# Undilated attention heads in blocks of 32 queries by 64 keys instead of 48 by 80, in a kernel of windowed attention and two feed-forward stages

## The reference, cut to what matters

```
scores = scale * q @ k.T                                   # B=4, H=8, S=576, D=64
mask_plain = (rel >= 0) & (rel < 32)                       # heads 0-3, rel = query - key
mask_dil   = (rel >= 0) & (rel < 128) & (rel % 4 == 0)     # heads 4-7
attn = exp(scores - max);  attn /= sum(attn) + 1e-9
x = attn @ v                                               # (4, 576, 512)
# feed-forward 1: token shift with mu_k, mu_r; r * (relu(xk @ w_k)^2 @ w_v), r = sigmoid(xr @ w_r)
# feed-forward 2: token mixing with w_tok1, w_tok2, channel mixing with w_ch1, w_ch2
```

## Time and profile before

| | us |
|---|---|
| median of 3 runs | 706.93 (706.69 to 707.06) |
| profiled execution | 707.65 |
| its span in the trace | 705.9 |
| TensorE matmuls busy | 698.6 |
| VectorE busy | 377.5 |
| ScalarE busy | 243.2 |
| GpSimd busy | 212.8 |

### The profile page before, as it was taken

How to read it: one execution, slowest core, us unless ns; L and a number is a source line. 1 busy time by engine, 2 the same in 40 slices (tenths; PEclk the granted TensorE clock), 3 DMA queues, 4 the chain that set the end, 5 groups by cost and what they waited for, 6 DMA issues and landing times.

```text
span 705.9 us, 13682 instructions
## 1 busy us (share of the span) xinstructions
PE 698.6 (99%) x5469; PEld 624.7 (88%) x5469; DVE 377.5 (53%) x609; ACT 243.2 (34%) x580; POOL 212.8 (30%) x228
## 2 busy tenths in 40 slices
PE   8999999999999999999999999999999999999997
PEld 8878999999999999999988888888788888888886
DVE  6689868687776777776872225321461225411121
ACT  3674563635445463636441122111231122211110
POOL 5584655756464664735045000000000000000000
PEclk9999999999999999999999999999999999999999
DMA  9941333222322220131912221303112121300011
GB/s 176 297 113 35 61 65 73 48 56 48 63 54 48 53 58 24 44 82 23 357 27 41 42 35 59 64 14 66 60 19 48 29 48 59 62 8 0 1 60 30
DMA packets 175695, 45.02 MB, mean 64 GB/s; under 512 B 163848, under 2 KB 168080, under 8 KB 175632
## 3 DMA queue, kind: packets, MB, share of 16 engines
q1 hardware_dynamic: 172192, 43.10, 27.3%
q10 hardware_dynamic: 3440, 1.05, 0.7%
HBM read 29.43 MB, written 4.72 MB: 48 GB/s over the span
## 4 chain that ended last, share of the span: by engine, by line
PE 96%; DVE 2%; issue 0%; ACT 0%; POOL 0%; DVEq 0%; POOLq 0%; ACTq 0%
PE bank L823 12%; PE bank L825 12%; PE bank L824 12%; PE tq L823 8%; PE tq L825 8%; PE tq L824 8%; PE s L1394 4%; PE s L1393 4%; PE s L1392 4%; PE bank L1393 3%; PE bank L1394 3%; PE bank L1392 3%; PE bank L711 3%; PE s L553 3%; PE bank L878 2%; PE bank L659 2%
## 5 line engine op out<-in xcount | busy, mean ns | idle before, releaser
L1384 DVE SCALAR_TENSOR_TENSOR h_lo<-bank,h_hi 128x512 fp32r<-128x512 f32 (+1 forms) x30 | 19.0, 637 | 100.7 <-ACT h_hi L1378 100.6
L1384 DVE SCALAR_TENSOR_TENSOR h_lo<-tq,h_hi 128x512 fp32r<-128x512 f32 (+1 forms) x30 | 18.9, 637 | 98.9 <-ACT h_hi L1378 98.9
L918 POOL TENSOR_TENSOR k_lo<-kr,k_hi 128x288 fp32r<-128x288 f32 x64 | 54.5, 855 | 23.2 <-ACT k_hi L914 22.5
L960 DVE RECIPROCAL rg<-rg 128x288 f32<-128x288 f32 x32 | 61.4, 1920 | 0.0
L1378 ACT ACTIVATE h_hi<-tq 128x512 fp32r<-128x512 f32 (+1 forms) x30 | 16.7, 556 | 118.7 <-PE bank L1394 97.0
L1378 ACT ACTIVATE h_hi<-bank 128x512 fp32r<-128x512 f32 (+1 forms) x30 | 16.7, 556 | 118.0 <-PE bank L1394 93.4
L823 PE MATMUL bank<-k_hi,WV_hi 128*128 128x288 f32 x184 | 56.1, 305 | 0.0
L824 PE MATMUL bank<-k_hi,WV_lo 128*128 128x288 f32 x184 | 54.3, 295 | 0.0
L825 PE MATMUL bank<-k_lo,WV_hi 128*128 128x288 f32 x184 | 54.1, 294 | 0.0
L599 POOL TENSOR_TENSOR sm<-sm,stat 128x640 f32<-128x640 f32 x24 | 30.6, 1277 | 76.8 <-DVE stat L591 76.8
L1394 PE MATMUL s<-C_hi,h_lo 128*128 128x512 f32 x120 | 47.5, 396 | 0.0
(11 more groups left out here) (218 smaller groups left out, 2016.8 us busy)
## 6 DMA issues: line engine op xcount, KB each, us to landing
C_raw<-in_moe_w_ch SPq DMA_DIRECT2D x6, 1024.0 KB, 10.9
urows<-blocks SPq DMA_DIRECT2D x64, 64.0 KB, 2.1
out_x<-urows SPq DMA_DIRECT2D x16, 256.0 KB, 2.1
vt<-in_v SPq DMA_DIRECT2D x40, 80.0 KB, 2.3
qraw<-in_q SPq DMA_DIRECT2D x128, 24.0 KB, 1.8
kraw<-in_k SPq DMA_DIRECT2D x128, 24.0 KB, 1.8
xraw<-blocks SPq DMA_DIRECT2D x48, 64.0 KB, 2.1
vt<-in_v SPq DMA_DIRECT2D x7, 320.0 KB, 3.9
```

Of the source, the lines that this page charges most:

```text
L918: e.tensor_tensor(lo, t, hi.bitcast(F32), ALU.subtract).then_inc(Z.lo_done, 1)
L960: e.reciprocal(t, t).then_inc(Z.r_done, 1)
L1384: e.scalar_tensor_tensor(lo, ps[:, 0:w], 0.0, hi.bitcast(F32), ALU.max, ALU.subtract).then_inc(Z.h2l_done, 1)
```

## The change

For even (plain) units a block becomes 32 queries by 64 keys. Four blocks fill 128 rows of the score tile, so a unit has 6 groups of 64 columns (128x384) instead of 8 of 80 (128x640), and two heads lie side by side in 128 columns. The score matmuls are 24 with 32 weight columns and 64 keys. `p_transpose` turns both heads of a group at once: 3 transposes of 128x128, one eviction of 128x384, into one bank. In `weighted_values` head h has its 64 keys in rows 64h to 64h + 63, so the two heads use the two row parts of TensorE: 24 matmuls of 64 rows, 64 columns, 32 queries. V of a plain unit comes in 8 DMAs (12 where j = 0) instead of 4. The sum of a plain unit gets its 1e-9 by an own small addition. The masks are built anew, V of unit 3 is loaded between the first and the second pair of WK loads, and waits are counted afresh. Dilated units keep their shapes.

```
+QP, KP = 32, 32 + WINDOW
+NP = SU // QP
         def v_loads(n):
-            return (2 if n == 3 else 1) if n % 2 else (8 if n == 2 else 4)
+            if n % 2:
+                return 2 if n == 3 else 1
+            return 8 if where(n)[1] else 12
         def load_v(n):
+                if not dil:
+                    for s in range(2):
+                        for h in range(2):
+                            vs = v[b, 2 * s + h, :, :]
+                            for u in range(2):
+                                t0 = SU * j + QP * u - WINDOW
+                                low = 0
+                                if t0 < 0:
+                                    e.dma_start(plain_v(n, slice(64 * h + WINDOW, 64 * h + KP), s)[:, 0, 0], vs[0:KP + t0]).then_inc(landed, 16)
+                                    low = 1
+                                e.dma_start(plain_v(n, slice(64 * h, 64 * h + KP), s)[:, u, low:],
+                                            vs[t0 + KP * low:t0 + SU, :].rearrange("(e p) d -> p e d", p=KP)).then_inc(landed, 16)
+                    return
         def scores(n):
+                if not dil:
+                    for s in range(2):
+                        for c in range(NP):
+                            g, a = divmod(NP * s + c, 4)
+                            for h in range(2):
+                                rows = slice(64 * h, 64 * h + 64)
+                                c0 = 512 * h + KP * g
+                                last = e.matmul(s2[QP * a:QP * (a + 1), c0:c0 + KP],
+                                                qT[rows, SU * s + QP * c:SU * s + QP * (c + 1)], keys(rows, s, c),
+                                                start=True, stop=True)
+                    last.then_inc(Z.s_done, 1)
+                    return
         def sums(n):
+                    e.tensor_reduce(st[:, 8:14], groups(n), AX.X, ALU.add).then_inc(Z.plain_sum, 1)
+                    e.wait_ge(Z.plain_sum, n // 2 + 1)
+                    e.tensor_tensor(st[:, 8:14], st[:, 8:14], st[:, 16:22], ALU.add).then_inc(Z.sum_done, 1)
         def p_transpose(n, h):
+                if n % 2 == 0:
+                    for g in range(3):
+                        last = e.transpose(ps[:, P * g:P * (g + 1)], sb[:, P * g:P * (g + 1)], ident[:, :])
+                    last.then_inc(Z.pa_done, 1)
+                    return
         def p_evict(n, h):
+                if n % 2 == 0:
+                    e.activation(p_buffer(n)[:, 0:2 * SU], p_bank(n, 0)[:, 0:2 * SU], ACT.Copy).then_inc(Z.pta_done, 1)
+                    return
         def weighted_values(n):
+                    if n % 2 == 0:
+                        for c in range(NP):
+                            for h in range(2):
+                                rows = slice(64 * h, 64 * h + 64)
+                                c0 = SU * s + QP * c
+                                last = e.matmul(o_[rows, c0:c0 + QP], plain_v(n, rows, s)[:, c % 2, c // 2],
+                                                p_buffer(n)[rows, c0:c0 + QP], start=True, stop=True)
+                        continue
         def loads():
-            steps = [..., load_v(0), load_v(1), load_v(2), load_v(3), load_mu(),
-                     load_weights1(w_k, WK, 0, 1, wk_in[0]), load_weights1(w_k, WK, 1, 1, wk_in[1]),
+            steps = [..., load_v(0), load_v(1), load_v(2), load_mu(),
+                     load_weights1(w_k, WK, 0, 1, wk_in[0]), load_weights1(w_k, WK, 1, 1, wk_in[1]), load_v(3),
```

More of the change, by code:

```diff
@@ L471, in dst @@
                         return raw_v(n, rows, h0, nh).rearrange("p (h c) -> p h c", h=nh)
[L472 to L480, removed]
+                    e.dma_start(dst(slice(skip, KB)),
+                                vs.rearrange("h (i r) d -> i h (r d)", r=DIL)[k0 + skip:k0 + KB]).then_inc(landed, 16)
             return dict(sync=sync)
@@ L562, in soft, with groups, per_group, spread @@
             return sm[i], stat[i]
-        def groups(t):
-            return t[:, :].rearrange("p (g x) -> p g x", g=8)[:, :, 0:KB]
+        def groups(n):
+            sb, _ = soft(n)
+            if n % 2:
+                return sb[:, :].rearrange("p (g x) -> p g x", g=8)[:, :, 0:KB]
+            return sb[:, 0:6 * KP].rearrange("p (g x) -> p g x", g=6)
+        def per_group(n, c0):
+            return soft(n)[1][:, c0:c0 + (8 if n % 2 else 6)]
+        def spread(n, c0):
+            return per_group(n, c0).unsqueeze(2).broadcast_to([P, 8, KB] if n % 2 else [P, 6, KP])
+        def turned(e, n):
+            if n % 2:
+                e.wait_ge(Z.pb_done, (n + 1) // 2)
+            else:
+                e.wait_ge(Z.pa_done, n + 1)
         def mask(n):
@@ L572, in vector @@
             def vector(e):
[L573 to L577, removed]
+                if n < 2:
+                    e.wait_ge(Z.const_done, N_MASKS if n else N_MASKS_P)
                 e.wait_ge(Z.s_done, n + 1)
                 if n >= 4:
-                    e.wait_ge(Z.pb_done, n - 1 if n >= 6 else n - 3)
@@ L649, in tensor @@
                 if n < 4:
[L650 to L651 removed]
+                    if n > 1:
+                        e.wait_ge(*((Z.ptb_done, 1) if h else (Z.pta_done, n - 1)))
+                elif n % 2 == 0:
+                    e.wait_ge(Z.pta_done, n)
+                    if n <= NPE:
+                        e.wait_ge(Z.ptb_done, n // 2)
+                elif h == 0:
+                    e.wait_ge(Z.pta_done, n)
                 elif n < NPE:
[L653 to L657 removed]
+                    e.wait_ge(Z.pta_done, n + 1)
+                elif n == NPE + 1:
+                    e.wait_ge(Z.q_done, NPE)
+                else:
+                    e.wait_ge(Z.ptb_done, (n - 1) // 2)
+                if n % 2 == 0:
[3 more added lines that the diff above has]
+                    return
                 for g in range(4):
@@ L1529, in _ @@
             e.memset(ident[:, :], 0.0).then_inc(Z.const_done, 1)
+            e.memset(masks_p[:, :], 0.0).then_inc(Z.const_done, 1)
             e.memset(masks[:, :], 0.0).then_inc(Z.const_done, 1)
-            e.wait_ge(Z.const_done, 2)
+            e.wait_ge(Z.const_done, 3)
             e.affine_select(out=ident[:, :], in_=ident[:, :], compare_op=ALU.not_equal, fill=1.0, base=0,
                             pattern=[[-1, P]], channel_multiplier=1).then_inc(Z.const_done, 1)
+            for a in range(4):
+                m = tiles(masks_p[QP * a:QP * (a + 1), :], 3)
+                e.wait_ge(Z.const_done, 4 + 2 * a)
+                e.affine_select(out=m, in_=m, compare_op=ALU.is_ge, fill=MASKED, base=WINDOW,
+                                pattern=[[0, 3], [-1, KP]], channel_multiplier=1).then_inc(Z.const_done, 1)
+                e.wait_ge(Z.const_done, 5 + 2 * a)
+                e.affine_select(out=m, in_=m, compare_op=ALU.is_ge, fill=MASKED, base=-1,
+                                pattern=[[0, 3], [1, KP]], channel_multiplier=-1).then_inc(Z.const_done, 1)
@@ L1535, in _ @@
+            for g in range(2):
+                first = masks_p[2 * QP * g:2 * QP * g + QP, KP * g:KP * (g + 1)]
+                e.wait_ge(Z.const_done, 12 + g)
+                e.affine_select(out=first, in_=first, compare_op=ALU.is_ge, fill=MASKED, base=-WINDOW,
+                                pattern=[[1, KP]], channel_multiplier=0).then_inc(Z.const_done, 1)
             for i, (lo_, hi_) in enumerate(((0, 64), (64, P))):
-                m = masks[lo_:hi_, :].rearrange("p (g x) -> p g x", g=5)
+                m = tiles(masks[lo_:hi_, :], 2)
+                e.wait_ge(Z.const_done, N_MASKS_P + 3 * i)
@@ L1547, in _ @@
+            e.wait_ge(Z.const_done, N_MASKS)
             main("gpsimd", e)
@@ L1559, in _ @@
             last.then_inc(Z.zeroed, 1)
-            for t in vts:
-                e.memset(t[0:WINDOW, :], 0.0)
+            for h in range(2):
+                for x in range(2):
+                    e.memset(plain_v(0, slice(64 * h, 64 * h + WINDOW), x)[:, 0, 0], 0.0)
+            e.memset(vts[1][0:WINDOW, :], 0.0)
             e.memset(X[:, :].rearrange("p (t n) -> p t n", n=XC)[:, :, 0:1], 0.0).then_inc(Z.zeroed, 1)
-            for t in sm:
+            for t in stat[0::2]:
+                e.memset(t[:, 16:22], 1e-9)
+            for t in sm[1::2]:
                 last = e.memset(t[:, :].rearrange("p (g x) -> p g x", g=8)[:, :, KB:KS], 1e-9)
```

106 lines of the change are left out of this document (61 added, 45 removed).

## The result

The changed kernel takes **712.64 us** (median of 6 runs, 710.04 to 713.84) beside 707.03 us before in the same runs: a ratio of 1.0076, interval 1.0058 to 1.0094. It is slower by 0.76%, where 697.3 us (695.5 to 705.0) was forecast. The profiled execution took 712.88 us, its span 711.1. The six runs differ by the clock granted to TensorE: the shortest, 710.04 us, had a mean of 0.997 of full speed, the longest, 713.84 us, of 0.990.

What follows compares the result with a forecast made beforehand. TensorE, busy 99% of the span, was taken as the bound; 8.4 us from the main phase and 1.2 from before 59 us make 9.6, so 707.65 becomes 698.0, a median of 697.3 us, range 695.5 to 705.0.

Steps and rivals of the forecast that it cites:

- Values: Weighted values of a plain unit on TensorE: from 1.07 to 0.83 us, 0.24 less per unit.
- I read the 29 ns as one load, serial within a row part: Weighted values: loads of different row parts overlap, so a pair of heads needs one load, 29 ns instead of 58.
- rival B: Weighted values: the two row parts do not run side by side, each instruction keeps 29 ns; 704.5 us; chance 0.15.
- the turns: Score-tile transposes on TensorE: three of 128 columns replace eight of 112, 0.33 us, 0.44 less per unit.
- Scores: Score matmuls of a plain unit: 6 rounds of eight tiles at 60 ns, 0.51 us instead of 0.71, 0.20 less.
- rival C: Scores: at most four score tiles together, 0.82 instead of 0.51 us over twelve units; 701.0 us; chance 0.14.
- rival E: Scores and values: each instruction has a floor of its own, deciding from 20 ns on; 717 us; chance 0.06.
- Tile shapes: Main phase, even units 10 to 22: values behind same-shaped scores save 0.07 us of filling each, 0.5 in all.
- Before 59 us: Prologue up to unit 5's turn: 1.4 us from units 0 and 2, 0.5 given back, 0.26 from unit 4: 1.2 gained.
- half a microsecond later is still hidden: Prologue, SP's queue: the last WK load lands by 23.8 us and is used after 26.07, so added issues stay hidden.
- The softmax in the prologue: VectorE steps before feed-forward 1: normalising unit 3 starts about 0.9 us earlier, with some 0.2 for the 1e-9 addition.
- SP in the main phase: SP's queue for plain units: 4 or 8 more issues, 2 to 4 us of queue each; no cost, a miss under 1 us.

Runs made afterwards that it cites:

- c: On a_mu_first, head 1's weighted values of plain units from 10 on write another PSUM bank, copy to X split: 713.33 us, ratio 1.0084.
- d: On a_mu_first, odd blocks' values from unit 10 on write crossed to a second bank, four array tiles in turn instead of two: 707.60 us, ratio 1.0004.
- g: On e, plain units from 10 on leave out half the keys of the scores and half the channels of the values: 701.49 us, one run.
- e: Changed kernel with V of a plain unit in 4 issues (8 where j = 0), V of unit 3 ahead of the weights again: 705.24 us, ratio 0.9972.
- h: On e with four-tile values, score matmuls run four blocks of one head, then four of the other: 700.23 us, one run.
- i: On e with four-tile values, score blocks in the order 0, 2, 1, 3: 700.90 us, ratio 0.9913.
- b_more_issues: Kernel before the change, with V of unit 2 in 16 issues of one head instead of 8 of two, same bytes: 709.64 us beside 707.43, one run.
- a_mu_first: Changed kernel with the two loads of mu ahead of V of unit 0 instead of behind V of unit 2: 712.01 us, ratio 1.0070.
- b_mu_late: Kernel before the change, with the two loads of mu behind the four WK loads: 710.53 us median, ratio 1.0062.

## Why the prediction was wrong

**Values: the step that failed is "I read the 29 ns as one load, serial within a row part".** The 58 ns of a pair were read as two loads of 29 ns, one after the other. As c, d and g show, they are the time in which one tile takes one load of 64 fp32 columns; two tiles do that side by side, and four do as well (d). The reading gives a load of 64 columns half the time it has: at the 0.81 ns a column of g, a single load is 52 of the 58 ns. The 27 ns of the forecast for 32 queries sent twice, from which its low end of 0.78 us comes, no run shows; the shortest pair of 32 queries took 28 ns (24 in 0.67 us, d). Both readings give 58 ns a pair before, since the pair had two tiles there too. After, the pair still has two tiles and still 64 weight columns, so it still costs 58 ns, and there are 24 pairs instead of 16: 24 x 58 = 1.39 us. With 0.13 of filling that is rival B's 1.52, which the right reading gives from the diff alone. The score rows, said to settle the matter, could not: in the earlier trace rows four tiles are visited in 70 ns, which allows 58 for each just as well as two times 29. The prediction called its own reading "the only reading with which both sets of rows agree", and that was false: every row shown fits both. With nothing to tell them apart the two deserved about the same chance, and the new block shape was the first place where they part.

In the window of the earlier trace rows TensorE was without a matmul for only 0.17 us, so what its queue saves there comes off the kernel's time. The measured terms of the main phase make up the 1.6 us: nine times 0.44 for the turns and 0.05 for the scores are 4.4; values lose seven times 0.30 and twice 0.45, 3.0; together 1.4.

**Scores: mis-sized, 0.66 for 0.51.** "I take 60" ns for a round of eight tiles. The 56 ns a round behind its bound of 0.49 us, and behind rival C's 0.82, no run shows; in e the first 32 starts, four rounds, take 0.25 us, 62 ns a round. The 48 instructions cost 0.66 us whatever their order, 14 ns each, and still 0.55 at half the keys. The first four rounds keep the forecast pace in e; what is lost comes behind them, where the starts are 17 ns apart. Why they slow isn't settled: neither sending alone (g), nor order (h, i) accounts for it. It isn't rival E, though, which needed 20 ns per instruction.

**Tile shapes: right in sign.** Values behind dilated scores of the same shape cost 0.15 us less than behind fp32r products; 0.07 was taken. The prediction has the values of unit n behind the scores of unit n - 3, the text on the order ahead of it behind those of unit n + 3. For units 10 to 22 they follow the scores of unit n + 1: the kernel puts them into slot `STARTS[n - 3] + 2`, and `STARTS` begins with unit 4. All three are of the other kind than unit n (L584 is ahead of L785 in the chain), so nothing in the sum moved.

**Before 59 us: the step that failed is "half a microsecond later is still hidden".** It priced the eight added issues at 0.44 to 0.5 us. They cost 0.60 each, and those of unit 2 rose from 0.44 to 0.61 too, some to over 1 us, so mu left 5.8 us later instead of 1.3 (3.7 less the 2.4 of unit 3). And it looked only at the end of the queue. It did not ask when mu and V of unit 3 are needed. mu was costed nowhere, and V of unit 3 only as queue time taken off ahead of the weights, not as a load that itself comes 8 us later. b_more_issues shows that even the cheap part, eight more issues at 0.42 to 0.45, was not hidden: 2.2 us.

**What no rival held: the clock.** It fell inside the wait of 2.9 us and stayed at 0.50 for 13.7 us. Of the 6.9 us lost, the wait is less than half.

**The softmax in the prologue** moved nearly as forecast: in e VectorE starts to normalise unit 3 at 20.12 us, 0.7 us earlier where 0.9 was forecast. The small addition for the 1e-9 takes 0.30 us in the changed kernel (L675), where "some 0.2" was taken. But the values of units 2 and 3 behind it run from 23.29 to 25.88 us, 2.59 us; before they ran from 24.21 to 26.07, 1.86. So feed-forward 1 starts 0.2 us earlier in e, not 1.4. Most of that is the term of the values again: those of unit 2 take 1.52 us instead of 0.93. Those of unit 3, which now follow another tile shape, take 1.07 instead of 0.93. SP in the main phase cost nothing, as said, and the masks, which were not tried apart, show in none of TensorE's waits: no wait of TensorE between 66 and 299 us is over 0.4 us.

In sum, of the 15.3 us between 697.3 and 712.6, 6.8 lie in the main phase (values 5.7, scores 1.35, which is about 0.2 more than the whole) and 8.1 before unit 5's turn; the rest, 0.4, is between the profiled execution and the median.

## What to carry to other kernels

Where a small fp32 matmul sends few columns, count what it costs by the columns of its weights and by how many different tiles of the array follow each other. Here 64 weight columns held a tile for 58 ns while 32 or 48 columns were sent; only the 80 keys of the old scores took longer (70 ns a round). With fewer queries in a block and the same number of tiles, a pair stayed at 58 ns. When a change adds DMA issues to a queue, go through every transfer behind them and ask when each is needed, the smallest first; one small late load can cost more than its wait. Here 6.9 us were lost around a wait of 2.9, with the clock at 0.50 for 13.7. An idea that measures slower may still be sound: with V in fewer issues and four tiles in turn the same blocks make the kernel 0.93% faster than it was.

## What the runs showed of the hardware

- Value matmuls with 64 fp32 weight columns follow each other on one tile every 58 ns, with 32 columns every 32 ns, at a granted clock of 1.00 (e and g); with 64 columns at 0.50 every 107 ns. Two and four tiles do so side by side: on four, 48 MATMUL rows took 0.67 us, 14 ns each (d). Products that send 512 columns start every 231 ns (before, 19 starts of L1392 to L1394 from 499.78 to 503.94 us, clock 1.00), 0.45 ns a column. At that rate 32 columns sent twice are about 29 ns, an estimate, so with 32 weight columns the load alone may be shorter than 32 ns.
- Two row parts writing different partitions of one bank are as fast as with two banks (1.37 us both, c).
- An issue on SP's queue for V of unit 2 cost 0.44 us in 80 rows of two heads, 0.42 in 80 rows of one head (b_more_issues) and 0.61 in 64 rows. For unit 0, earlier in the queue, it was 0.55 to 0.79 in 80 rows and mostly 0.60 in 64 or 32. In each of these prologues one to three issues took 1.2 to 1.9 us. These runs don't show what the price depends on; it isn't the bytes, since 32 rows of one block cost as much as 64 rows of three.
- The granted clock fell to 0.50 inside a wait of 2.9 us and stayed there for 13.7 us (changed kernel); inside one of 4.9 us it fell for 6.8 us (a_mu_first). With a wait of 1.3 us (b_mu_late), and with waits of 1.0 and 0.5 us (b_more_issues), the profiled runs kept 1.00, but five of ten runs of the first kind had a mean of 0.990 to 0.993.
